# Weight sums, hidden tiles ahead, transposes and ScalarE's order in a fused attention, experts and MLP kernel

## The reference

```python
# attention with decay: q, k, v are 2 x 8 x 576 x 64
scores = q @ k.T / sqrt(64)
ret = (scores * gamma_h ** (i - j) for i >= j, else 0) @ v        # per head
x = ret as 1152 tokens x 512
# four experts, w1 512 x 1024, w2 1024 x 512, all of them used for each token
p = probs / (probs.sum(-1) + 1e-9)
x = sum over e of p[:, e] * (relu(x @ w1[e]) @ w2[e])
# MLP, w_in 512 x 2048, w_out 2048 x 512
h = x @ w_in
out = (h * tanh(softplus(h))) @ w_out
```

## Time and profile before

| | |
|---|---|
| median of three runs | 665.88 us (665.01 to 666.33) |
| the profiled execution | 667.55 us, its span 665.8 us |
| mean granted TensorE clock | 0.982 of full speed |
| busy share of the span | TensorE 96%, VectorE 50%, GpSimd 43%, ScalarE 39% |
| w_hi of one weight tile, ScalarE, mean | 619 ns, 96 of them |
| transfers | 46.26 MB, mean 69 GB/s |

### The profile page before, as it was taken

The page is one execution under the profiler, slowest core; times in us unless marked ns, Lnnn a source line. Parts: engine busy times, 40 slices in busy tenths (PEclk is TensorE's granted clock), DMA queues, the critical chain, the costliest instruction groups (busy, mean ns, idle before and its releaser), DMA issues.

```text
span 665.8 us, 9870 instructions
## 1 busy us (share of the span) xinstructions
PE 641.9 (96%) x3812; PEld 571.9 (86%) x3813; DVE 336.1 (50%) x588; ACT 260.1 (39%) x515; POOL 286.8 (43%) x247
## 2 busy tenths in 40 slices
PE   8999789999999999999999999995899999899998
PEld 5788679999899999899999999985789999799996
DVE  4644732323132223132232143366778799998784
ACT  2454423432233332333422234344454555465441
POOL 4557634433535533635334643334213456642220
PEclk9899979999999999999999999997799999999999
DMA  7855211312202322112322221311000121001011
GB/s 255 305 175 171 81 46 64 96 64 64 64 33 64 100 75 63 48 45 82 98 62 64 65 64 64 94 48 47 1 1 1 36 59 33 1 0 48 1 48 48
DMA packets 22814, 46.26 MB, mean 69 GB/s; under 512 B 2608, under 2 KB 2928, under 8 KB 22768
## 3 DMA queue, kind: packets, MB, share of 16 engines
q1 hardware_dynamic: 22480, 45.46, 22.1%
q10 hardware_dynamic: 288, 0.17, 0.1%
HBM read 43.26 MB, written 2.36 MB: 69 GB/s over the span
## 4 chain that ended last, share of the span: by engine, by line
PE 81%; DVE 11%; ACT 3%; issue 2%; POOL 2%; ACTq 0%; DVEq 0%; POOLq 0%
PE bank L510 25%; PE bank L511 25%; PE bank L512 25%; DVE m_w L936 3%; PE bank L464 2%; PE bank L504 1%; DVE m_c L942 1%; DVE m_a L934 1%; DVE m_n L945 1%; PE bank L666 1%; DVE h_lo L913 1%; ACT m_r L777 1%; POOL w_lo L406 1%; PE bank L468 1%; ACT w_hi L379 1%
## 5 line engine op out<-in xcount | busy, mean ns | idle before, releaser
L406 POOL TENSOR_TENSOR w_lo<-w_raw,w_hi 128x512 fp32r<-128x512 f32 x96 | 128.2, 1338 | 132.6 <-ACT w_hi L379 132.5
L510 PE MATMUL bank<-w_hi,h_hi 128*128 128x512 f32 x432 | 170.3, 394 | 1.8 <-DVE acc_sb L925 1.8
L512 PE MATMUL bank<-w_hi,h_lo 128*128 128x512 f32 x432 | 170.7, 395 | 0.0
L511 PE MATMUL bank<-w_lo,h_hi 128*128 128x512 f32 x432 | 170.6, 395 | 0.0
L1046 POOL TENSOR_TENSOR m_t<-m_w,m_r 128x384 f32<-128x384 f32 x48 | 55.2, 1150 | 128.0 <-ACT m_r L779 128.0
L890 DVE TENSOR_TENSOR h_act<-part,bank 128x384 f32<-128x384 f32 x64 | 35.5, 554 | 146.1 <-PE bank L512 145.8
L512 PEld LDWEIGHTS bank<-w_hi,h_lo 128*128 128x128 f32 x432 | 81.6, 189 | 17.6
L510 PEld LDWEIGHTS bank<-w_hi,h_hi 128*128 128x128 f32 x432 | 81.8, 189 | 13.0 <-DVE acc_sb L925 2.2
L511 PEld LDWEIGHTS bank<-w_lo,h_hi 128*128 128x128 f32 x432 | 81.7, 189 | 10.8
L748 ACT ACTIVATE h_hi<-h_act 128x384 fp32r<-128x384 f32 x64 | 33.6, 525 | 120.0 <-DVE h_act L890 120.0
L401 POOL TENSOR_TENSOR ws<-ws_f,ws 128x1024 fp32r<-128x1024 f32 x16 | 38.3, 2394 | 91.3 <-ACT ws L375 91.3
(11 more groups left out here) (89 smaller groups left out, 1137.5 us busy)
## 6 DMA issues: line engine op xcount, KB each, us to landing
w_raw<-in_weights SPq DMA_DIRECT2D x128, 256.0 KB, 2.7
qkv<-in_chunks SPq DMA_DIRECT2D x18, 512.0 KB, 4.4
out<-acc_sb SPq DMA_DIRECT2D x2, 768.0 KB, 3.7
out<-acc_sb SPq DMA_DIRECT2D x3, 256.0 KB, 2.1
consts<-in_consts ACTq DMA_DIRECT2D x1, 146.0 KB, 3.8
ident<-in_consts SPq DMA_DIRECT2D x1, 64.0 KB, 4.0
consts<-in_consts SPq DMA_DIRECT2D x1, 34.0 KB, 4.0
p_nat<-in_probs ACTq DMA_DIRECT2D x1, 18.0 KB, 4.0
```

Of the source, the lines that this page charges most:

```text
L406: pool.tensor_tensor(w_lo[:, layer, x], w_raw[:, r % RAW], w_hi[:, layer, x].bitcast(F32), ALU.subtract).then_inc(s_wl, 1)
L510: pe.matmul(out, w[0], x[0], start=first, stop=False, **more)
L511: pe.matmul(out, w[0], x[1], start=False, stop=False, **more)
L512: return pe.matmul(out, w[1], x[0], start=False, stop=last, **more)
```

## The change

It has four parts. The first weight-sum job goes from turn 17 to turn 15, and the w2 tiles around it move: 0 to 2 stand in turns 12 to 14, 3 to 5 in turns 16 to 18; ScalarE does its part of the sum job one turn later than GpSimd, ahead of that turn's other job. `AHEAD` becomes 4; the tables of steps are written anew for it. The eight transposes of blocks 1 and 2 stand at n = -2 to 1 and 3 to 6, which is m = 2 to 5 and 7 to 10 (before m = 2 to 5 and 6 to 9). ScalarE's order changes in product stages (the copies of P6 and P7 ahead of the first job, later jobs behind C22 and C21) and in MLP steps (`second_hi` right behind exp).

```diff
-AHEAD = 6
+AHEAD = 4
-TURN_IN = {-4: (1, 0), -3: (1, 1), -2: (1, 2), -1: (1, 3), 0: (2, 0), 1: (2, 1), 2: (2, 2), 3: (2, 3)}
+TURN_IN = {-2: (1, 0), -1: (1, 1), 0: (1, 2), 1: (1, 3), 3: (2, 0), 4: (2, 1), 5: (2, 2), 6: (2, 3)}
...
-    for u in range(4):
+    for u in range(3):
+        add(IN_TURN, 12 + u, "w2", 0, u)
+    add(IN_TURN, 15, "s", 0, 0)
+    for u in range(3, 6):
         add(IN_TURN, 13 + u, "w2", 0, u)
-    add(IN_TURN, 17, "s", 0, 0)
-    add(IN_TURN, 18, "w2", 0, 4)
-    add(IN_TURN, 18, "w2", 0, 5)
...
-    for n, job in zip((-6, -6, -5, -4, -3, -2), (("w1", 6), ("w1", 7), ("w2", 4), ("w2", 5), ("w2", 6), ("w2", 7))):
+    for n, job in zip((-4, -3, -2, -1, 0, 1), (("w1", 6), ("w1", 7), ("w2", 4), ("w2", 5), ("w2", 6), ("w2", 7))):
         add(IN_STEP, n, job[0], e, job[1])
     for u in range(UNITS):
-        add(IN_STEP, 11 + u, "w1", e + 1, u)
+        add(IN_STEP, 13 + u, "w1", e + 1, u)
     for u in range(UNITS):
-        add(IN_STEP, 18 + u, "w2", e + 1, u)
+        add(IN_STEP, 20 + u, "w2", e + 1, u)
...
                 if c > 0:
                     first_hi(c - 1)
+                for job in IN_TURN.get(c - 1, ()):
+                    if JOBS[job][0] == "s":
+                        job_hi(act, job)
                 for job in IN_TURN.get(c, ()):
-                    job_hi(act, job)
+                    if JOBS[job][0] != "s":
+                        job_hi(act, job)
...
                     keep(s, 0, P1)
                     sum_hi(s, C11)
+                    keep(s, 1, P6)
+                    keep(s, 2, P7)
                     for job in todo[0:1]:
                         job_hi(act, job)
-                    keep(s, 1, P6)
-                    for job in todo[1:2]:
-                        job_hi(act, job)
-                    keep(s, 2, P7)
-                    for job in todo[2:3]:
-                        job_hi(act, job)
                     sum_hi(s, C22)
-                    for job in todo[3:4]:
+                    for job in todo[1:3]:
                         job_hi(act, job)
                     sum_hi(s, C21)
-                    for job in todo[4:]:
+                    for job in todo[3:]:
                         job_hi(act, job)
...
                 if m < MT:
                     mish_exp(m)
+                if n in TURN_IN:
+                    second_hi(*TURN_IN[n])
                 if 0 <= m - 2 < MT:
                     hi(m - 2)
                 if m < MT:
                     mish_inv(m)
-                if n in TURN_IN:
-                    second_hi(*TURN_IN[n])
```

## The result

The changed kernel takes 646.85 us in the median of four runs (643.83 to 649.03), the kernel before 665.44 beside it (663.70 to 666.33). The ratio is 0.9721, with a 95% interval of 0.9675 to 0.9766: faster, by 18.6 us where 19.4 were forecast. The profiled execution took 649.03 us, with a span of 647.2.

What follows compares the result with a forecast made beforehand. TensorE's work plus two disturbances, at the front and the MLP entrance, was taken as the bound. Gains of 9.1 and 10.3 summed to 19.4 us, giving 646.5 us from the median 665.88; range 641.5 to 653.5.

Steps and rivals of the forecast that it cites:

- the front: Waits and low clock around 60 to 92 us, before P6 and P7: 9.1 us gained in all.
- the entrance: MLP entrance, 450 to 490 us: earlier second_hi and four tiles ahead gain 10.3 us, bounds 7 and 12.
- (e): MLP steps: second_hi behind mish_exp lets second_lo follow m_w; turn(1,1) at 452.45 instead of 454.07, steps without conversion 3.6 us.
- (a): Front: sum job two turns earlier, so P1's copy is done before P6 is due; gain 1.94 us.
- (b): Product stages: copies of P6 and P7 ahead of ScalarE's first job end the wait before P7; gain 4.52 us.
- (c): Front: without the 4.52 us idle before P7 the clock does not fall; gain 3.05 us.
- (d): Turn 12: two conversions there may push the attention turns; 0.4 us lost, bounds 0 to 2.
- Rival B: MLP entrance: ScalarE takes over the wait, loop stays near 5.12 us; gain there 6.9, in all 649.9; chance 0.13.
- D: Rival, MLP entrance: both GpSimd instructions stop VectorE in full, 1.3 us more in m = 3, 4, 5; 650.4; chance 0.06.
- (f): MLP entrance: four tiles ahead give TensorE projections from m = 4, only 0.3 us idle behind turn(1,2).
- (g): Later MLP steps: less depth leaves h_lo 1.9 us of cover, 0.3 at the end; cost 0, bounds 0 and 2.
- S: Rival, m = 24 to 31: four tiles too few, TensorE waits for h_lo and the clock falls; 679.8 us; chance 0.03.

Runs made afterwards that it cites:

- e1: On the kernel before, only the first weight-sum job moved to turn 15, with the w2 tiles around it: 662.41 us, ratio 0.9959.
- e2: On the kernel before, only ScalarE's order in product stages changed, copies of P6 and P7 ahead of the first job: 660.62 us, ratio 0.9932.
- e3: On the kernel before, only second_hi moved right behind exp in MLP steps, still six tiles ahead: 657.46 us, ratio 0.9893.
- e7: On the changed kernel, w2 conversions 4 to 7 of the first MLP half in m = 6 to 9 instead of 2 to 5: 644.74 us, ratio 0.9670.
- e6: The changed kernel with six tiles ahead instead of four, transposes and conversions at the same hidden tiles: 648.87 us, ratio 0.9743.
- e4: On the kernel before, only four tiles ahead with the change's tables, second_hi still last in ScalarE's step: 662.24 us, ratio 0.9948.
- e5: The changed kernel with three tiles ahead instead of four, transposes and conversions at the same hidden tiles: 650.83 us, ratio 0.9772.
- e8: e7 plus the second half's eight w2 conversions one step later, so no step has two: 641.08 us, ratio 0.9636.

## Why the prediction was right

The stretches give 9.82 + 9.73 = 19.55 against 19.4 worked out; the 1.00 us that separates them from the measured 18.6 lies in the attention's start, which the change doesn't touch. The mechanism is right in both places. That the totals agree this closely is in part luck: the front came out 0.7 better than its 9.1, the entrance 0.6 worse than its 10.3, and inside (e) two prices were wrong and cancelled.

(a) Right. Less the 1.00 of start, the sums began at 57.85 (58.0 worked out), the low half was ready at 64.5 (64.7), the copy of P1 done at 75.2 (75.7), P6 started at 76.8 without a wait. e1 shows that the move does this by itself.

(b) Right: e2 and the profile after have no wait before P7. The conversions that moved behind C22 and C21 cost nothing that shows: no wait stands between 65 and 439 us.

(c) Right, 3.05: the clock stays full; in e1, with 3.12 us of wait left, it still fell. With (a) and (b) 9.5 were expected without (d) and 9.82 came; the 0.3 more is in no term of the sum.

(d) Too careful: 0.4 was taken, 16.53 - 16.52 = 0.01 measured.

(e) Right: turn(1,1) came 1.61 us earlier relative to turn(1,0) (4.34 against 5.95; 1.62 worked out), the next 4.64 later (4.65). Rival B, that ScalarE takes over the wait, did not come: e3 alone gained more than B gave with both edits. But the 4.65 was met in part by luck. The sum took VectorE's time from a step of before in which the conversion held up `m_c`, 1.1 us more than its usual 0.55:

```profile
454.37 1.62 DVE L942 SCALAR_TENSOR_TENSOR m_c<-m_r,m_t 128x384 f32<-128x384 f32 x1
```

In the new order `m_c` is not held up (0.55). The conversion meets `m_a` (0.85 us in the entrance's timeline above, 0.35 before), and `m_t` meets `m_n` (1.25, before 0.56): 1.2 us more. So steps with a conversion came out as worked out, and those without one did not, as e7 shows (4.14 instead of 3.6).

D had half of this: `m_t` does hold VectorE up now, by 0.7 us. It did not come as a whole, because the two GpSimd instructions of that step (1.08 and 1.60 us) lengthen it from 3.6 to 4.64 and not by their sum. The Trainium skill's rule on the shared access ("SBUF — State Buffer", Who interferes with whom) fits the pairs of instructions: `m_n`, with two SBUF inputs, is drawn out beside `m_t`, and `h_act`, which reads a bank and one SBUF tile, keeps its 0.56 us beside `w_lo`. Adding up all of GpSimd's time overstates the price, since instructions like `h_act` go on beside it.

(f) Right: with `second_hi` moved, the depth takes away 1.2 us of waits (e6), and no turn waits behind turn(1,2). Worked out for e4 alone it was mis-sized, 4.9 against 2.34; 1.5 of the gap is a clock fall elsewhere.

(g) Right: no projection waits for `h_lo` with four tiles, and e5 shows that three is one too few (2.6 us). The late wait stayed and moved to m = 28.

The clock at the entrance: 1.0 was taken, 1.6 came. That is not what separates the 10.3 of the sum from the 9.73 measured, since the waits came out smaller than taken, 3.8 against 4.0 + 0.3. From the end of hidden(3) (443.65 - 1.75 = 441.90) to the end of turn(2,3) (476.71 + 0.3) the kernel after takes 35.1 us for 7 x 2.12 + 7 x 0.3 + 6 x 2.04 = 29.2 of work. So 5.9 are lost where 5.3 were taken: 3.8 of waits, 1.6 of clock, 0.5 in neither. The 15.6 lost before is a difference of the same kind and holds such a rest too (9.1 of waits and 5.9 of clock make 15.0). The sum subtracted from it a loss that was added up from waits and clock alone.

What the argument against S rested on, full clock around the wait of 1.80 us, is true of that execution and not of the kernel, as the last section shows. It did not decide anything here.

## What to carry to other kernels

Where an engine takes its instructions in order, look at what stands ahead of the short copy that the bounding engine waits for; moving the copy ahead of a job that waits for a third engine gave 7.6 us (e2), and one more place of the same kind 7.5 (e3). Spread background work so that no step has two pieces of it: the lag that one double step made (m = 24) was paid four steps later (m = 28) as a wait with another name. Reordering one engine's queue also changes which of its neighbour's instructions meet; a price read from a step of the old order holds for the old meetings only. And cut the executions that are compared at the same instructions; unchanged stretches then agreed within some hundredths of a us in most executions and within 0.5 in all, where medians moved by 2 to 3 without a reason in the change. A clock fall that comes only sometimes (below) still has to be looked for inside the stretch and taken off.

## What the runs showed of the hardware

The start of the attention differs from execution to execution, whatever the kernel: the last output of the attention started between 59.39 and 64.68 us in thirteen profiled executions (59.39 to 64.03 among the eight kernels whose attention is the same), and the front behind it agreed within 0.02 us in all eight kernels that have both front edits. In the kernel after, the clock was at 0.50 in the windows from 24 to 28 us, in e8, which has the earliest start, at 1.00 there. I did not look for the cause.

The late wait of 1.76 to 1.91 us before the output banks stands in nine profiled executions. The clock fell to 0.50 behind it in three (e4, e5, e6; 1.5 to 1.7 us of loss each) and stayed full in six. So an idle time of this length sometimes costs as much again, and a single profile does not tell how often.
